# Chunked attention and two MoE layers in one kernel: PSUM banks for the first tile's odd chunks, an earlier rounding of q and k, row sums on VectorE, column sums on GpSimd

## What is computed

```python
scores = scale * np.matmul(q_c, k_c.transpose(0, 1, 2, 4, 3))       # chunks of 64 rows
attn = np.exp(scores - scores.max(-1, keepdims=True))
x = np.matmul(attn / (attn.sum(-1, keepdims=True) + 1e-09), v_c)    # -> (4608, 512)
h = x @ w_in                                                        # (4608, 2048)
g = s * np.maximum(h, 0) ** 2 + b
x2 = g @ w_out                                                      # (4608, 512)
# second layer: rows with x2 @ w_skip > 0 go to one of 8 experts (argmax of x2 @ w_gate),
# out = x2 + p * relu(x2 @ w1[e]) @ w2[e]; the others stay x2
```

## Time and profile before

| | |
|---|---|
| three runs | 1446.62, 1449.09 (median), 1450.95 us |
| the profiled execution | 1447.19 us |
| its span in the profile | 1445.3 us |
| PE products busy | 1351.7 us, 94% |
| PE weight loads | 1179.8 us, 82% |
| VectorE | 823.5 us, 57% |
| ScalarE | 845.7 us, 59% |
| GpSimd | 310.1 us, 21% |
| opening loop | 0 to 54.6 us |
| tile 0 with column sums | 54.6 to 147.6 us |
| tiles 1 to 10 | to some 941 us |
| tile 11, end of routing, experts | to the end |

### The profile page before, as it was taken

One profiled execution on the slowest core, in us unless ns is written; L12 is line 12 of the kernel. 1 busy time (PEld: TensorE's weight loads), 2 busy tenths in 40 slices (PEclk: granted clock), 3 DMA queues, 4 the chain that ended last, 5 costly groups with the idle time before them and its releaser, 6 DMA issues.

```text
span 1445.3 us, 22903 instructions
## 1 busy us (share of the span) xinstructions
PE 1351.7 (94%) x7032; PEld 1179.8 (82%) x7033; DVE 823.5 (57%) x2058; ACT 845.7 (59%) x2483; POOL 310.1 (21%) x262
## 2 busy tenths in 40 slices
PE   4699999999999999999999999999388899999998
PEld 3688989888888989888888889898366777888887
DVE  3464666766666666667666666655356645332332
ACT  6796686758676776857685867744154544222221
POOL 4221122222221212222222212200112122111111
PEclk9999999999999999999999999999699999999999
DMA  5132210312021212112021202032555741111110
GB/s 208 70 132 96 77 56 30 103 28 92 30 91 29 99 34 70 62 32 99 30 92 32 88 30 99 12 103 74 161 174 207 243 146 46 43 44 44 43 43 25
DMA packets 61463, 116.28 MB, mean 80 GB/s; under 512 B 11705, under 2 KB 20921, under 8 KB 61217
## 3 DMA queue, kind: packets, MB, share of 16 engines
q1 hardware_dynamic: 40816, 73.51, 15.2%
q10 hardware_dynamic: 14416, 27.79, 5.6%
q0 software_dynamic: 6112, 13.56, 2.8%
HBM read 90.49 MB, written 27.08 MB: 81 GB/s over the span
## 4 chain that ended last, share of the span: by engine, by line
PE 39%; ACT 27%; DVE 15%; issue 12%; DMA 5%; POOL 1%; DVEq 1%; ACTq 0%; SPq 0%; POOLq 0%
ACT soft L785 11%; PE y_ps L712 9%; PE h_ps L594 9%; PE h_ps L699 8%; PE y_ps L608 8%; DVE products L1003 4%; ACT qk_hi L761 4%; DMA wide<-x_rows,got 3%; DVE probs_t_lo L944 3%; DVE row_max L950 3%; ACT g_hi L761 2%; ACT scratch L821 2%; ACT scratch L817 2%; ACT rows_t_hi L761 2%; DMA got<-table 2%
## 5 line engine op out<-in xcount | busy, mean ns | idle before, releaser
L594 PE MATMUL h_ps<-rows_t_hi,weights_lo 128*128 128x384 f32 x768 | 261.1, 340 | 8.2 <-issue 5.8
L594 PE MATMUL h_ps<-rows_t_hi,weights_hi 128*128 128x384 f32 x768 | 260.3, 339 | 0.0
L594 PE MATMUL h_ps<-rows_t_lo,weights_hi 128*128 128x384 f32 x768 | 258.7, 337 | 0.0
L608 PE MATMUL y_ps<-weights_hi,g_lo 128*128 128x512 f32 x576 | 230.9, 401 | 0.4 <-DVE g_lo L982 0.3
L608 PE MATMUL y_ps<-weights_hi,g_hi 128*128 128x512 f32 x576 | 227.2, 395 | 0.0
L608 PE MATMUL y_ps<-weights_lo,g_hi 128*128 128x512 f32 x576 | 226.4, 393 | 0.0
L1003 DVE CUSTOM_DVE_ANT_0 products<-scratch,wide 128x512 f32<-128x512 f32 x297 | 204.2, 687 | 5.1
L464 POOL TENSOR_TENSOR qk_lo<-qk_raw,qk_hi 128x768 fp32r<-128x768 f32 x66 | 121.7, 1844 | 392.1 <-ACT qk_hi L761 392.1
L982 DVE TENSOR_TENSOR g_lo<-scratch,g_hi 128x384 fp32r<-128x384 f32 x192 | 124.3, 647 | 130.8 <-ACT g_hi L761 127.8
L817 ACT ACTIVATE scratch<-h_ps 128x384 f32<-128x384 f32 x192 | 94.5, 492 | 172.3 <-PE h_ps L594 167.8
L785 ACT ACTIVATE soft<-s_ps,row_bias 64x64 f32<-64x64 f32 x576 | 171.2, 303 | 3.2
(11 more groups left out here) (147 smaller groups left out, 2447.4 us busy)
## 6 DMA issues: line engine op xcount, KB each, us to landing
qk_raw<-in_qk SPq DMA_DIRECT2D x66, 384.0 KB, 3.0
expert_raw<-in_w ACTq DMA_DIRECT2D x32, 512.0 KB, 4.9
scratch<-in_w ACTq DMA_DIRECT2D x21, 512.0 KB, 5.3
out<-scratch SPq DMA_DIRECT2D x12, 768.0 KB, 3.9
x_rows<-scratch SPq DMA_DIRECT2D x12, 768.0 KB, 5.5
v_raw<-in_v SPq DMA_DIRECT2D x66, 128.0 KB, 2.1
expert_raw<-in_w SPq DMA_DIRECT2D x11, 512.0 KB, 3.7
wide<-in_w_out SPq DMA_DIRECT2D x7, 512.0 KB, 4.2
```

The costliest lines, as they stand in the source:

```text
L594: mm = pe.matmul(h_ps[f % 2][:, 0:TOK], w[:, f // PAIR, kt, fs], x[:, z, kt, :], start=kt == 0 and n == 0, stop=kt == KT - 1 and n == 2)
L608: mm = pe.matmul(y_ps[t][:, :], g[:, f % 2, ts], w[:, f, :], start=f == 0 and n == 0, stop=f == FT - 1 and n == 2)
```

## The change

Five things are edited.

1. In the first tile (chunks 0 to 5) the odd chunks use three other PSUM banks, the y banks, for scores, transposed probabilities and products with v. PE's waits there look two chunks back instead of one.
2. Stage A of chunk c stands at 2c - 1 (0 for chunk 0) instead of 2c. The orders inside a half-step are new: ScalarE C, g_hi, A, D, B (at f = 15: D first, then C, g_hi, A, B), VectorE C, B, g_lo, D (at f = 15: D first). In the opening loop ScalarE goes D, A, C, B instead of D, C, A, B, and GpSimd A, C instead of C, A. For chunks 0 to 5 GpSimd makes v_hi itself. At f = 14 PE's D of the last chunk stands in the middle of h(15)'s products, ahead of the ranking products.
3. The exponentials no longer give row sums; VectorE sums the 128x256 probabilities in one reduction ahead of the eps.
4. The column sums of w_out are made from the raw w_out pieces: GpSimd adds them up in float32, 15 additions of 128x512, into `bias`, in tile 0's odd half-steps; PE then makes one float32 product with a matrix of ones.
5. SyncE also waits for these additions before it reloads an odd buffer, and its loads are reordered: in the looped tiles the first v load comes ahead of the first q, k load.

```diff
@@ banks
+        def s_of(n):
+            return y_ps[0] if odd_first(n) else s_ps
+        def av_of(n):
+            return y_ps[1] if odd_first(n) else av_ps
+        def turned_probs(n):
+            return (y_ps[2] if odd_first(n) else t_ps)[:, 0:2 * P].rearrange("p (J n) -> p J n", J=2)
@@ stages
-                for name, at in (("D", 2 * c + 4), ("C", 2 * c + 3), ("B", 2 * c + 1), ("A", 2 * c)):
+                for name, at in (("D", 2 * c + 4), ("C", 2 * c + 3), ("B", 2 * c + 1), ("A", max(2 * c - 1, 0))):
@@ SyncE
+                if job >= RAWS and (job - RAWS) % 2:
+                    sp.wait_ge(column_step, job - RAWS)
                 load_raw(sp, job)
...
-            for slot in range(-3, 2 * CPT + 1):
-                if slot + 8 < JOBS:
-                    load_raw_after(slot + 8)
-                if slot >= 1 and slot % 2:
-                    load_qk(CPT + (slot - 1) // 2 + SLOTS, (slot - 1) // 2)
-                if slot >= 2 and slot % 2 == 0 and slot < 2 * CPT:
-                    load_v(CPT + slot // 2)
+            load_raw_after(RAWS)
+            load_raw_after(RAWS + 1)
+            load_raw_after(RAWS + 2)
+            load_qk(CPT + SLOTS, 0)
+            load_raw_after(RAWS + 3)
+            load_raw_after(RAWS + 4)
+            for c in range(1, CPT):
+                load_qk(CPT + c + SLOTS, c)
+                for job in range(RAWS + 2 * c + 3, min(RAWS + 2 * c + 5, JOBS)):
+                    load_raw_after(job)
+                load_v(CPT + c)
+            sp.wait_ge(column_step, JOBS - 1)
             sp.wait_ge(raw_done, JOBS - EARLY)
...
             def tile_loads(t, last=False):
+                load_v(CPT * t)
                 for c in range(CPT):
                     if c + SLOTS < CPT or not last:
                         load_qk(CPT * t + c + SLOTS, c)
-                    load_v(CPT * t + c)
+                    if c > 0:
+                        load_v(CPT * t + c)
@@ GpSimd
+            pool.memset(products[:, 0:P], 1.0).then_inc(consts, 1)
...
             def lo_of_v(n):
+                src = v_raw[:, :]
+                if isinstance(n, int) and n < CPT:
+                    src = first_v[n]
+                    pool.wait_ge(first_v_in[n], 16)
+                    if n > 0:
+                        pool.wait_ge(av_done, n)
+                    pool.tensor_copy(v_hi[:, :], src).then_inc(v_hi_done, 1)
                 pool.wait_ge(v_hi_done, n + 1)
...
+            def column_sums(job):
+                pool.wait_ge(raw_in[job], 16)
+                r = raw[job % RAWS]
+                if job == 1:
+                    pool.tensor_tensor(bias[:, :], r[:, 0:DM], r[:, DM:2 * DM], ALU.add).then_inc(column_step, 1)
+                else:
+                    for n in range(2):
+                        pool.wait_ge(column_step, job - 2 + n)
+                        pool.tensor_tensor(bias[:, :], bias[:, :], r[:, n * DM:(n + 1) * DM],
+                                           ALU.add).then_inc(column_step, 1)
...
+                    if isinstance(i, int) and i == 0 and f % 2 and f + 2 < JOBS:
+                        column_sums(f + 2)
@@ PE
+            def before_last(n):
+                return 1 if isinstance(n, int) and n < CPT else 0
...
-                    if not (isinstance(n, int) and n == 0):
-                        pe.wait_ge(exp_done, n)
+                    if not (isinstance(n, int) and n < 2):
+                        pe.wait_ge(exp_done, n - before_last(n))
...
-                    if f + 1 < FT:
+                    if attend and f == 2 * CPT + 2:
+                        into_h(i, f + 1, z, range(KT // 2))
+                        attention("D", CPT * (i + 1) + CPT - 1, CPT - 1)
+                        into_h(i, f + 1, z, range(KT // 2, KT))
+                    elif f + 1 < FT:
                         into_h(i, f + 1, z)
...
-                pe.wait_ge(raw_done, JOBS - EARLY)
+                pe.wait_ge(column_step, JOBS - 1)
                 pe.wait_ge(exp_done, 2 * CPT)
-                pe.wait_ge(ones_set, 1)
-                for f in range(FT):
-                    for n, w in enumerate((w_out_lo, w_out_hi)):
-                        mm = pe.matmul(s_ps[:, :], v_hi[:, 0:P], w[:, f, :], start=f == 0 and n == 0,
-                                       stop=f == FT - 1 and n == 1)
-                mm.then_inc(sums_done, 1)
+                pe.matmul(s_ps[:, :], products[:, 0:P], bias[:, :], start=True, stop=True).then_inc(sums_done, 1)
@@ ScalarE
-                            last = act.activation(probs[xs, c % 2, h, :], s_blocks[xs, h, x, :], ACT.Exp,
-                                                  bias=row_bias[xs, h:h + 1], scale=SCALE, accum_out=row_sum[xs, h:h + 1])
+                            last = act.activation(probs[xs, c % 2, h, :], s_blocks(n)[xs, h, x, :], ACT.Exp,
+                                                  bias=row_bias[xs, h:h + 1], scale=SCALE)
...
+                    order = "DCgAB" if f == FT - 1 else "CgADB"
@@ VectorE
                     dve.wait_ge(exp_done, n + 1)
+                    dve.tensor_reduce(row_sum[:, :], probs[:, c % 2, :, :], AX.X, ALU.add).then_inc(sum_done, 1)
+                    dve.wait_ge(sum_done, n + 1)
...
+                    order = "DCBg" if f == FT - 1 else "CBgD"
```

More of the change, by code:

```diff
@@ L498, in _ @@
             for step in range(-1, CPT + 2):
-                for stage, c in first_chunks(step, ("C", "A")):
+                for stage, c in first_chunks(step, ("A", "C")):
                     if stage == "A":
@@ L583, in split_by_then, with into_h @@
                     pe.wait_ge(raw_done, jobs - EARLY)
-            def into_h(i, f, z):
+            def into_h(i, f, z, part=range(KT)):
                 if f == 0:
@@ L591, in into_h @@
                 fs = slice(f % PAIR * P, (f % PAIR + 1) * P)
-                for kt in range(KT):
+                for kt in part:
                     for n, (w, x) in enumerate(((w_in_lo, TH1), (w_in_hi, TL1), (w_in_hi, TH1))):
@@ L636, in tile @@
                         rank(i - 1)
[L637 removed]
+                    if attend and f != 2 * CPT + 2:
                         for stage, c in stages(f):
@@ L779, in attention @@
                     act.wait_ge(row_bias_done, n + 1)
-                    if not (isinstance(n, int) and n == 0):
-                        act.wait_ge(probs_done, n)
                     for x in range(2):
@@ L791, in attention @@
                         ys = slice(64 * y, 64 * y + 64)
-                        last = keep(p_hi[ys, :, y, :], turned_probs[ys, :, :])
+                        last = keep(p_hi[ys, :, y, :], turned_probs(n)[ys, :, :])
                     last.then_inc(probs_hi, 1)
-                    if first:
-                        act.wait_ge(first_v_in[c], 16)
-                    else:
+                    if not first:
                         act.wait_ge(v_in, 16 * (n - CPT) + 16)
-                    keep(v_hi[:, :], first_v[c] if first else v_raw[:, :]).then_inc(v_hi_done, 1)
+                        keep(v_hi[:, :], v_raw[:, :]).then_inc(v_hi_done, 1)
                 if stage == "D":
@@ L848, in _ @@
             for step in range(-1, CPT + 2):
-                for stage, c in first_chunks(step, ("D", "C", "A", "B")):
+                for stage, c in first_chunks(step, ("D", "A", "C", "B")):
                     attention(stage, c, c, 0, 0)
@@ L854, in _ @@
             tile(0, 0, True, False)
-            act.activation(v_hi[:, 0:P], ident[:, :], ACT.Identity, scale=0.0, bias=1.0).then_inc(ones_set, 1)
             act.wait_ge(scalars_in, 32)
```

88 lines of the change are left out of this document (46 added, 42 removed).

## The result

The changed kernel takes 1428.87 us (median; 1427.66 to 1431.54) against 1447.86 of the kernel before beside it: ratio 0.9868, 95% interval [0.9846, 0.9891], so 1.3% faster, 19.0 us. The prediction said 1429.7. Its sum was made against one profiled execution, so the comparison by stage is more telling than the total.

| | before | after | gained in the stage | predicted |
|---|---|---|---|---|
| first h product | 54.60 | 53.26 | 1.34 | 0.65 |
| column product(s) | 138.06 | 133.60 | 3.12 | 3.0 |
| second h of tile 1 | 147.59 | 136.54 | 6.59 | 6.8 |
| end of tile 11 (first routing transposes) | 1007.73 | 989.27 | 7.41 | 7.0 |
| sum | | | 18.46 | 17.5 |

A forecast was written before the change was run, and what follows sets the result against it. PE was taken as busy nearly throughout, with ScalarE also nearly full in tile 0. Gains of 0.65 + 3.0 + 6.8 + 7.0 = 17.5 us off 1447.19 gave 1429.7 us; range 1420 to 1441.

The forecast's parts named there:

- The signs named ahead: Whole kernel: no qk_lo waits beyond half-step 1, pairs 10.1 to 10.3 in tile 0, 10.0 looped, opening rounds about 7.3.
- Opening: First six chunks, second PSUM banks and new ScalarE and GpSimd orders: 0.65 us gained, ends 2.0 gained and 0.4 lost.
- v_hi ... together taken as 0.75: Opening round on GpSimd: v_hi copy 0.36 to 0.73 plus 0.1 to 0.3 wait on itself, taken as 0.75 us.
- the second banks do not shorten the round: Opening: GpSimd's chain makes a round 7.3 us, longer than 6.87; the banks shorten only the first two rounds.
- no PE time: Row sums on VectorE: reduction of 0.45 us lies before a product due half a step later, costing PE nothing.
- the exponentials two half-steps earlier end some 0.7 sooner: Tile's end: sooner exponentials cut the 1.1 us stall of h(15) on p_lo to 0 to 0.4.
- Part 3: q, k rounded half a step earlier: looped tiles gain 10 x (1.3 - 0.6) = 7.0 us, ends 17 and -4.
- Half-step 1: Looped tiles: chunk 0's rounding comes behind square and g_hi, so scores wait; -0.6 us per tile, between -0.4 and -0.8.
- Tile's end: Last av product inside h(15): possible 0.4 us from earlier x, offset by routing steps; zero, ends +0.4 and -0.9 per tile.
- Column sums: End of tile 0: 32 products of 7.49 us replaced by one float32 product of 0.66; 6.8 us gained, ends 6.5 and 7.25.
- which fits: Looped tiles: VectorE's pair of half-steps becomes 7.05 + 0.45 + 1.85 = 9.35 us busy of 10.0.
- Rival (c): Looped tiles: VectorE becomes the bound, qk_lo stopping even half-steps' gate product; pairs 11.6 instead of 10.45, 1494 us; chance 0.05.

The follow-up runs named there:

- the version with late rounding and x first: Changed kernel with q, k rounded at 2c again and attention output ahead of the gate in odd half-steps on ScalarE and VectorE: 1427.47 us.
- the version with the reads back and the early rounding: Changed kernel with row sums back on ScalarE through accumulator reads, VectorE's reduction removed, q, k rounding still early: 1441.31 us.
- the slow version: Changed kernel with q, k rounded at 2c again, ahead of g_hi, attention output still behind the gate: 1466.34 us, ratio 1.0112 to the kernel before.

## Why the prediction was right, point by point

**The total** came out 0.8 us from the median. Three of four stages are within 0.5 us, but some of the reasons were wrong, and a match this close is in part luck: in the loop 1.6 us lost to the clock stand against about as much more won at the waits. The signs named ahead are there: no score product waits for qk_lo beyond half-step 1, pairs are 10.0 to 10.2 in tile 0 but for one of 10.55 that waits for g_lo, two g_lo rows there last 1.46 and 1.52, and nothing waits for the gate load.

**Opening: mechanism right, one term too big.** The step said "v_hi ... together taken as 0.75"; it measured 0.39, and 0.08 from its end to v_lo, where the working had 0.1 to 0.3 for the wait on itself from no row. Hence rounds of 6.94 and not 7.3, chunk 5's scores at 40.60 (41.9 predicted), the last av at 49.88 (50.55), and 1.34 us for 0.65. That "the second banks do not shorten the round" was borne out. The 1.34 is the low end: in this trace VectorE's addition of eps at 45.98 starts inside GpSimd's v_lo and lasts 0.70 instead of 0.17, on the path to the last transposes. In the five traces of the same opening in which it does not, the first h product starts at 52.61 to 52.79, 0.5 to 0.65 sooner.

**Row sums: "no PE time" was the costliest error.** The working had the missing piece: "the exponentials two half-steps earlier end some 0.7 sooner", which keeps p_lo in time at the tile's end. It was booked as a condition of Part 3 and given no price; taking it away costs 10 us, 7.8 of them at the tiles' ends.

**Earlier rounding: the size right, the cause not the only one.** 1.3 us per tile were won (three pairs of 10.00 instead of 10.45), but I gave them to the rounding's new place. With the old place and x ahead of the gate nobody waits either. Two rows of the kernel before show what the loop hung on there, the transposes of one chunk and the qk_lo of the next:

```profile
173.76 0.38 PE L565 MATMUL t_ps<-ident,soft 128*128 128x128 f32 x2
...
181.49 1.85 POOL L464 TENSOR_TENSOR qk_lo<-qk_raw,qk_hi 128x768 fp32r<-128x768 f32 x1 [5.27 <-ACT qk_hi L761]
```

From the transposes to the end of qk_lo it took 9.58 us (173.76 to 183.34), through the probabilities' split, the row maxima, the exponentials (2.6 us with their reads, from 177.45 to 180.03) and the rounding. The scores stood 0.76 ahead of the transposes (173.00), so a pair of 10.00 wanted qk_lo after 9.24: too late by 0.34. In the version with late rounding and x first the same way took 8.59 (173.73 to 182.32), as the exponentials take 1.84, and the scores stand 0.14 behind the transposes, so that qk_lo has 10.14. By these rows the shorter exponentials alone would be enough (an estimate: 9.58 - 0.73 = 8.85 against 9.24), and so would PE's new order alone (9.58 against 10.14), which the prediction left out; neither was run alone. The earlier rounding is enough too, as the version with the reads back and the early rounding has pairs of 10.0, though with PE's new order. They are three changes that each end the same wait by these numbers, and I counted one; no run brings the old pairs of 10.45 back, so which of them counts is argued from rows and not shown. In tile 0 the earlier rounding does pay: from the first h product to the column product it takes 80.3 us, and 82.6 with the late rounding and x first (both orders differ between the two).

**Half-step 1: right.** -0.6 was predicted, between -0.4 and -0.8; h takes 2.66 instead of 2.11 there and the scores 0.82 instead of 0.71, 0.66 in all. A tile gains 1.33 in half-steps 7, 9 and 11, 0.09 in 3 and 5 (which the working had at nothing), 0.09 at its end, and loses 0.66: 0.85, times 10 is 8.5. With 0.4 in the loop's tops and the rest, less the 1.6 of the clock, that is the 7.41 measured. So the forecast of 7.0 was nearer to the result than its terms: the clock, which it did not have, made up for the difference.

By the Trainium skill's rule (SBUF — State Buffer, Who interferes with whom), that the lock holds whoever comes first, I had put -0.8 beside the -0.6. The direction that the trace of before did not show is there now: the qk_lo that starts at 141.26 inside a gate product (140.96 to 141.65) takes 2.07 instead of 1.84, where a full wait for that product would make it 2.23, and the longest of all takes 2.26. The trace agrees with the rule; the price, -0.66, was between the two.

**Tile's end: zero, right**, as 5.34 stands against a mean of 5.43 (5.63 and 5.23), but the reason for a gain that the working left open, "an earlier x", does not exist: x_lo still keeps h(0) waiting 0.40.

**Column sums: 6.59 for 6.8.** The float32 product holds PE for 0.46, and the y products behind it take 2.48 instead of 2.04, nearly all of it between the first and the second (134.06 and 134.69): 0.90 in all, where I had 0.66 from transposes. The Trainium skill (FP8 and Floating Point Precision) has four passes for true fp32, by estimate 0.94 at 0.23 a product; the trace comes closer to that than to my row.

**VectorE: 9.35 forecast, 9.05 seen, "which fits".** It does in this order, and a small change of order brings out pairs of 11.1 and 1466 us. Rival (c), VectorE as the bound, had 0.05. It did not come true here, but its idea, a queue on VectorE held up by qk_lo, is what the slow version has; there qk_lo stops g_lo in the odd half-step and not the gate product in the even one.

## What to carry to other kernels

An engine is not safe because it is under 100% busy: ask in which order its queue stands when what it waits for comes late, since a ring through three queues can set the period well before the engine is full (here at 8.7 to 9.4 of 11.1 us). Price what an edit makes shorter even where nobody waits for it now, as another edit may live off that slack; and when a single edit is taken back, ask which of the others now stands without it. Before paying for new buffers, look at which engine closes the round; here, with the banks in place, a swap of two stages on GpSimd brought the opening's end 4.4 us forward, where the three more banks under the first order had brought 0.4. And read a gain by stage from the trace before adding up totals: one half-step at a lowered clock was as large as some of the terms.

## What the runs showed of the hardware that was not expected

VectorE's gate product takes 0.69 us alone and up to 2.34 beside GpSimd's qk_lo; qk_lo takes up to 2.26 instead of 1.84, v_lo up to 1.30 instead of 0.74. In the changed kernel, minimum, median and maximum in ns, first and last start:

```profile
L1051 DVE CUSTOM_DVE_ANT_0 products<-scratch,wide x297: 679/692/2337, 139.5 to 979.2; 128x512 f32<-128x512 f32 x149
...
L491 POOL TENSOR_TENSOR qk_lo<-qk_raw,qk_hi x66: 1831/1840/2257, 62.2 to 895.5; 128x768 fp32r<-128x768 f32 x66
...
L503 POOL TENSOR_TENSOR v_lo<-v_raw,v_hi x66: 737/738/1297, 75.2 to 913.8; 128x256 fp32r<-128x256 f32 x66
```

VectorE's row_max and p_lo, which read PSUM, kept their 0.86 beside GpSimd's qk_lo, and so did x_lo in the version with late rounding and x first. A tiny instruction is stretched too: the addition of eps to 128x4 row sums takes 0.17 us alone, and up to 1.08 when it starts inside one of GpSimd's subtractions or additions (1.08 in the version with chunk 0's rounding first). In the changed kernel the one at 45.98 ends 0.03 after v_lo, at 46.68, and one at 68.99 ends 0.03 after the end of a qk_lo, at 69.71.

A turn of the loop costs PE 1.0 to 2.2 us at its top, in every version. After the one that ends at 609.43 in the changed kernel the mean granted clock from 605 to 615 was 0.83, as part of that stretch ran at 1.2 and not 2.4 GHz, and the half-step took 5.81 instead of 4.25. Seven of the twelve changed versions show one such half-step, 1.5 to 1.6 us longer, each behind a turn's top that took 1.96 to 2.2 us more than elsewhere. The same window in the version with chunk 0's rounding first has a gap of 2.2 and a clock of 1.00, and the kernel before had gaps of up to 2.0 without it. So the length of the gap alone does not decide, and what does was not tried.
